# The first two chunks reordered, and layer norm's weight folded into W1: one change to a linear-attention, MLP and expert kernel

## The reference, cut to what matters

```python
for t in range(S):
    cur = np.einsum('bhd,bhe->bhde', u[None] * kt, vt)
    y[:, :, t] = np.einsum('bhd,bhde->bhe', rt, state + cur)
    state = w[None, :, :, None] * state + np.einsum('bhd,bhe->bhde', kt, vt)
```

```python
xn = (x - mu) / np.sqrt(var + 1e-06) * g_ln
ch = np.maximum(xn @ w_ch1, 0.0) @ w_ch2
return x + ch
```

## Time and profile before

| | us |
|---|---|
| median of 3 runs | 412.55 (412.34 to 412.64) |
| the profiled execution's own time | 412.14 |
| its span, first to last instruction | 410.3 |
| PE busy in the span | 399.5 (97%) |
| DVE, ACT, POOL busy | 227.3, 162.5, 120.1 |
| mean granted clock of TensorE | 0.987 of full speed |

### The profile page before, as it was taken

How to read it: one execution, slowest core, us unless ns; L and a number is a source line. 1 busy time by engine, 2 the same in 40 slices (tenths; PEclk the granted TensorE clock), 3 DMA queues, 4 the chain that set the end, 5 groups by cost and what they waited for, 6 DMA issues and landing times.

```text
span 410.3 us, 8140 instructions
## 1 busy us (share of the span) xinstructions
PE 399.5 (97%) x2761; PEld 369.4 (90%) x2761; DVE 227.3 (55%) x455; ACT 162.5 (40%) x300; POOL 120.1 (29%) x111
## 2 busy tenths in 40 slices
PE   8999999999999999999999999999999999999992
PEld 7999999999999999999999965679999999999982
DVE  7566954532542452344466856878853665638340
ACT  5456223232321321223234126356754672555530
POOL 2675280650162054000000400712331133114221
PEclk9699999999999999999999999999999999999998
DMA  7994310420330033140002848499894549111111
GB/s 225 344 290 125 104 40 6 143 79 19 99 106 19 19 102 102 45 149 2 19 22 64 285 137 287 147 314 313 291 371 155 180 129 370 66 30 41 27 41 41
DMA packets 32631, 54.87 MB, mean 134 GB/s; under 512 B 3261, under 2 KB 20323, under 8 KB 32592
## 3 DMA queue, kind: packets, MB, share of 16 engines
q1 hardware_dynamic: 30288, 48.07, 36.0%
q0 software_dynamic: 2304, 6.30, 5.0%
HBM read 49.64 MB, written 5.51 MB: 134 GB/s over the span
## 4 chain that ended last, share of the span: by engine, by line
PE 91%; DMA 3%; ACT 2%; DVE 1%; SPq 1%; issue 1%; POOL 0%; DVEq 0%; POOLq 0%
PE bank L940 6%; PE bank L856 6%; PE bank L857 6%; PE bank L858 6%; PE bank L942 6%; PE bank L946 6%; PE bank L894 5%; PE bank L1236 5%; PE bank L1208 5%; PE bank L1244 5%; PE bank L1240 5%; PE bank L1212 5%; PE bank L1215 5%; PE bank L1225 3%; PE bank L868 3%; PE bank L1137 3%
## 5 line engine op out<-in xcount | busy, mean ns | idle before, releaser
L652 ACT ACTIVATE parts<-bank 128x512 fp32r<-128x512 f32 x36 | 21.5, 597 | 85.1 <-PE bank L946 85.1
L1394 DVE SCALAR_TENSOR_TENSOR parts<-bank,parts 128x512 fp32r<-128x512 f32 x36 | 24.8, 690 | 45.2 <-ACT parts L652 45.1
L856 PE MATMUL bank<-parts 128*128 128x384 f32 x144 | 49.0, 341 | 0.0
L858 PE MATMUL bank<-parts 128*128 128x384 f32 x144 | 48.2, 335 | 0.0
L857 PE MATMUL bank<-parts 128*128 128x384 f32 x144 | 48.2, 334 | 0.0
L732 ACT ACTIVATE parts<-stage (+1 forms) x32 | 46.1, 1485 | 2.5 <-DMA stage<-in_w 2.3
L1702 DVE TENSOR_TENSOR parts<-stage,parts x24 | 41.1, 1756 | 5.3 <-ACT parts L732 4.5
L595 POOL DMA_INDIRECT out_y<-late x14 | 20.4, 1460 | 77.8 <-DVE late L1733 77.8
L940 PE MATMUL bank<-xnT_hi,parts 128*128 128x256 f32 x216 | 40.5, 296 | 0.5 <-DVE parts L1353 0.5
L942 PE MATMUL bank<-xnT_hi,parts 128*128 128x256 f32 x216 | 37.6, 283 | 0.0
L946 PE MATMUL bank<-xnT_lo,parts 128*128 128x256 f32 x216 | 37.6, 283 | 0.0
(11 more groups left out here) (239 smaller groups left out, 808.9 us busy)
## 6 DMA issues: line engine op xcount, KB each, us to landing
stage<-in_w SPq DMA_DIRECT2D x36, 768.0 KB, 7.5
stage<-in_w_ch SPq DMA_DIRECT2D x6, 768.0 KB, 9.3
arena<-in_k_t SPq DMA_DIRECT2D x12, 224.0 KB, 3.0
arena<-in_r_t SPq DMA_DIRECT2D x12, 224.0 KB, 2.9
arena<-in_k_rows SPq DMA_DIRECT2D x12, 192.0 KB, 2.8
arena<-in_v_rows SPq DMA_DIRECT2D x12, 192.0 KB, 3.4
x_rows<-stage SPq DMA_DIRECT2D x12, 192.0 KB, 1.9
arena<-in_r_rows SPq DMA_DIRECT2D x10, 192.0 KB, 2.6
```

Of the source, the lines that this page charges most:

```text
L652: act.activation(hT_hi[:, 2 * q:2 * q + 2, :].rearrange("p a t -> p (a t)"), bk[6 + q % 2][:], ACT.Relu).then_inc(h_hi_ready, 1)
L856: pe.matmul(out_, a_lo, b_hi, start=start, stop=False)
L858: return pe.matmul(out_, a_hi, b_hi, start=False, stop=stop)
L1394: dve.scalar_tensor_tensor(hT_lo[:, at, :].rearrange("p a t -> p (a t)"), bk[6 + q % 2][:], 0.0, hT_hi[:, at, :].rearrange("p a t -> p (a ...
```

## The change

Seven edits:

1. The decays of chunk 0 are made pair by pair (`decays_by_pair`): eight instructions of 128 columns instead of two of 512, each waiting only for the table of its own pair. `scores(0)` waits for one pair at a time, by the new semaphore `s_pair`.
2. The load of the first constants (identity and mask) is issued ahead of kT and rT of chunk 1, and on DVE `masked(0)` now stands ahead of chunk 1's decays (`second_decays`).
3. On TensorE `scores(1)` moves behind `from_scores(0)`, and matmuls on zeros are placed between the narrow ones: 2, 2, 4, 2 and 4 of them, where 16 stood in one block.
4. The factor -g_ln goes from `turned` into `round_piece` and `rest_of_piece` of pieces 0 to 2. Those now take three instructions each, one for a block of 128 features, and `turned` takes one instruction per chunk on ACT and one on DVE, in every group.
5. Piece 0's lo goes from POOL to DVE, ahead of `turned(0)`. `lo_p` is gone; everything counts on `lo_v`.
6. `ngcol` is made by POOL between `ends(0)` and `ends(1)`.
7. On ACT `centre(0)` and `turned(0)` move ahead of piece 1, and in group 0 every further piece comes one place later: piece 2 behind hidden 0, piece 3 behind hidden 1, piece 4 behind hidden 2, piece 5 behind the decay of chunk 3's state. The decay of chunk 2's state now stands ahead of piece 4.

```diff
@@ sync
             for u in range(2):
                 sp.dma_start(kT[u], k_t[u]).then_inc(s_turned[u], 16)
                 sp.dma_start(rT[u], r_t[u]).then_inc(s_turned[u], 16)
-            sp.dma_start(cst[:, 0:P + C], consts[:, 0:P + C]).then_inc(s_const, 16)
+                if u == 0:
+                    sp.dma_start(cst[:, 0:P + C], consts[:, 0:P + C]).then_inc(s_const, 16)
@@ gpsimd
             ends(0)
+            pool.wait_ge(s_g, 16)
+            pool.tensor_scalar(ngcol[:], gcol[:], -1.0, None, ALU.mult).then_inc(s_ng, 1)
             ends(1)
             diagonal(0)
-            pool.wait_ge(s_g, 16)
-            pool.tensor_scalar(ngcol[:], gcol[:], -1.0, None, ALU.mult).then_inc(s_ng, 1)
             diagonal(1)
-            first_piece(0)
-            first_piece(1)
@@ scalar
             def round_piece(i):
                 act.wait_ge(s_piece[i], 16)
-                act.activation(piece_at(i, 0), piece_stage(i), ACT.Copy).then_inc(hi_done, 1)
+                if i >= KD:
+                    act.activation(piece_at(i, 0), piece_stage(i), ACT.Copy).then_inc(hi_done, 1)
+                    return
+                if i == 0:
+                    act.wait_ge(s_ng, 1)
+                for k in range(KD):
+                    mm = act.activation(piece_at(i, 0)[:, k, :], piece_stage(i)[:, k, :], ACT.Copy, scale=ngcol[:, k:k + 1])
+                mm.then_inc(hi_done, 1)
...
-                    for k in range(KD):
-                        i = act.activation(xnT_hi[:, k, u * P:(u + 1) * P], bk[u][:, k * P:(k + 1) * P], ACT.Copy,
-                                           scale=ngcol[:, k:k + 1])
-                    i.then_inc(xnT_hi_ready, 1)
+                    act.activation(xnT_hi[:, :, u * P:(u + 1) * P],
+                                   bk[u][:, 0:DM].rearrange("p (k t) -> p k t", k=KD), ACT.Copy).then_inc(xnT_hi_ready, 1)
@@ tensor
             def scores(c, u, banks):
...
                 for p in range(NP_):
+                    if isinstance(c, int) and c == 0:
+                        pe.wait_ge(s_pair, p + 1)
...
             coefs(0, bk[3])
-            scores(1, 1, bk[6:8])
+            keep_warm(1, 5)
             for u in range(2):
                 pe.wait_ge(s_rows[u], R_FIRST)
             from_scores(0, 0, bk[4], scT[0], True)
+            keep_warm(1, 5)
+            scores(1, 1, bk[6:8])
             coefs(1, bk[0])
+            keep_warm(2, 5)
             from_scores(1, 1, bk[5], scT[1], True)
...
             gain(0, 0, bk[3])
+            keep_warm(1)
             turn_xn(0, lambda: gain(1, 1, bk[2]))
-            keep_warm(8)
+            keep_warm(2)
             pe.wait_ge(s_gw, 16)
@@ vector
+            def decays_by_pair():
+                dve.wait_ge(s_turned[0], T_LOADS)
+                for p in range(NP_):
+                    dve.wait_ge(s_wk, p + 1)
+                    k = dve.tensor_tensor(kT[0][:, p, :], kT[0][:, p, :], w_k[:, p, :], ALU.mult)
+                    if p == NP_ - 1:
+                        k.then_inc(kdec_ready, 1)
+                    dve.wait_ge(s_wr, p + 1)
+                    dve.tensor_tensor(rT[0][:, p, :], rT[0][:, p, :], w_r[:, p, :], ALU.mult).then_inc(s_pair, 1)
...
             def rest_of_piece(i):
                 dve.wait_ge(hi_done, i + 1)
...
+                for k in range(KD):
+                    x = dve.scalar_tensor_tensor(piece_at(i, 1)[:, k, :], piece_stage(i)[:, k, :], ngcol[:, k:k + 1],
+                                                 piece_at(i, 0)[:, k, :].bitcast(F32), ALU.mult, ALU.subtract)
+                x.then_inc(lo_v, 1)
...
-            first_decays(0)
+            decays_by_pair()
             raw_products(0)
-            first_decays(1)
             dve.wait_ge(s_const, 16)
             masked(0, bk[0:2], scT[0])
+            second_decays()
+            first_coefs(0, bk[3])
             raw_products(1)
-            first_coefs(0, bk[3])
...
             mean(0, 1)
-            dve.wait_ge(s_ng, 1)
+            rest_of_piece(0)
             turned(0)
             rest_of_piece(1)
```

More of the change, by code:

```diff
@@ L673, in group @@
                 if first:
-                    round_piece(3)
+                    round_piece(2)
                 else:
@@ L685, in group @@
                 if first:
-                    round_piece(5)
+                    round_piece(4)
                 hidden(g, range(3, 4))
                 decay(g * 2 + 3, 1)
+                if first:
+                    round_piece(5)
                 hidden(g, range(4, NHP))
@@ L711, in _ @@
             round_piece(0)
+            centre(0)
+            turned(0)
             round_piece(1)
-            centre(0)
-            act.wait_ge(s_ng, 1)
-            turned(0)
             act.wait_ge(s_eps, 1)
             deviation(0)
-            round_piece(2)
             group(0)
@@ L860, in scores @@
             def scores(c, u, banks):
-                pe.wait_ge(kdec_ready, c + 1)
-                pe.wait_ge(rdec_ready, c + 1)
+                if not isinstance(c, int) or c > 0:
+                    pe.wait_ge(kdec_ready, c + 1)
+                    pe.wait_ge(rdec_ready, c + 1)
                 if not isinstance(c, int) or c >= 2:
@@ L1384, in turned @@
                     at = slice(u * P, (u + 1) * P)
-                    for k in range(KD):
-                        i = dve.scalar_tensor_tensor(xnT_lo[:, k, at], bk[u][:, k * P:(k + 1) * P], ngcol[:, k:k + 1],
-                                                     xnT_hi[:, k, at].bitcast(F32), ALU.mult, ALU.subtract)
-                    i.then_inc(xnT_ready, 1)
+                    dve.tensor_tensor(xnT_lo[:, :, at], bk[u][:, 0:DM].rearrange("p (k t) -> p k t", k=KD),
+                                      xnT_hi[:, :, at].bitcast(F32), ALU.subtract).then_inc(xnT_ready, 1)
             def hidden(g, pairs):
```

47 lines of the change are left out of this document (18 added, 29 removed).

## The result

The changed kernel is slower. Its median of 6 runs is 418.75 us (417.75 to 420.17), against 412.44 (411.13 to 414.30) of the kernel before in 6 runs: ratio 1.0155, 95% interval 1.012 to 1.0191. The forecast was 411.15, with a range up to 412.6, and gave "slower" a chance of 0.15. It had the sign wrong.

The account below looks back on a forecast made before the run. TensorE, busy in 97% of the span, was taken as the bound. Gains of 0.9 us at `scores(2)` and 0.5 at q = 4 made -1.4, so 412.55 became 411.15; own range 410.7 to 411.6, full range 410.3 to 412.6.

Parts of the forecast that it names:

- 0.9 us at `scores(2)`: Chunk 2's scores on TensorE, behind POOL's two products, were to start at 26.0 instead of 26.88: -0.9 us.
- 0.5 at q = 4: In group 0, TensorE's 0.53 us wait for piece 2's lo was to go, with the state decay ahead of piece 4.
- just clear of 23.33: DVE's lo of piece 1 was to run from 21.3 to 23.2, before kT of chunk 2 lands at 23.33.
- paragraph on the clock: If the low stretch stays, hi is there at 21.6 and group 0 starts at 21.7: 0.2 us lost.
- POOL held again: Rival at POOL's first product for chunk 2: 2.01 us again, 0.7 of the gain goes, 411.85; chance 0.12.
- The first chunks gain nothing up to there.: Start-up: `from_scores(0)` at 9.55 instead of 10.70, the gain given back, x of chunk 1 at 16.4 to 16.6.
- It matters only if a half-speed stretch comes after 20.95: TensorE's clock ahead of group 0: half speed there was to cost only 0.2 us against the sum.
- The slower rival: Clock falls at 21 or later, after waits for `wg` and POOL; 6.8 us half speed, +1.4, 413.95; chance 0.14.
- What it set against itself: Against the slower case: at the trace's end TensorE idled from 402.5, the clock fell only at about 406.7.
- kT of chunk 2: Transfer that POOL's chunk 2 products wait for; taken to land at 23.33, as before the change.
- The start of group 0 that it forecast, 20.95: TensorE was to start group 0 behind router weights `wg`, landed at 20.93, instead of at 22.39.
- The fold costs nothing in the later groups: Cheaper `turned` runs under output matmuls while TensorE has no wait from 40 to 240 us: 0, with 0.1 either way.

Follow-up runs that it names:

- e2: Changed kernel with the fold taken back: a piece's hi and lo one instruction each, `turned` three; 415.57 us, ratio 1.0075.
- e7: Kernel before with only ACT's order in group 0 changed: decay of chunk 2's state ahead of piece 4, piece 5 later; 412.08 us, ratio 0.9998.
- e13: Changed kernel with chunk 1's scores and decays back in their old order and piece 1's hi early; 412.01 us, ratio 0.9993.
- e16: Changed kernel with piece 1's lo made in six instructions of 256 columns instead of three of 512; 422.06 us, ratio 1.0227.
- e1: Changed kernel with one wait added: POOL begins chunk 2 only when DVE has made piece 1's lo; 416.06 us, ratio 1.005.
- e4: Changed kernel with ACT rounding piece 1 ahead of `centre(0)`, as before the change; 416.52 us, ratio 1.0089.
- e6: Kernel before with edits 4 to 7 alone (fold, piece 0's lo on DVE, `ngcol` earlier, ACT's new order); 414.84 us, ratio 1.0041.
- e12: Kernel before with edits 4 to 7 alone, but ACT's hi of piece 1 ahead of `centre(0)`; 414.11 us, ratio 1.0005.
- e15: Kernel before with DVE's order alone changed: chunk 1's decays behind `masked(0)`, `first_coefs(0)` ahead of `raw_products(1)`; 418.82 us, ratio 1.0152.
- e14: Kernel before with one move on TensorE alone: `scores(1)` behind `from_scores(0)`; 414.45 us, ratio 1.0043.
- e10: Kernel before with edits 1 to 3, but the 16 zeros left in one block; 415.76 us, ratio 1.0066.
- e5: Kernel before with edits 1 to 3 alone (decays by pair, mask first, `scores(1)` later, zeros spread); 416.55 us, ratio 1.0076.
- e3: Changed kernel with 30 matmuls on zeros on TensorE behind chunk 2's scores, where it waited before q = 2; 419.08 us, ratio 1.0133.
- e8: Changed kernel with 48 instead of 14 matmuls on zeros in the first chunks; 418.3 us, ratio 1.0126.
- e9: Kernel before with only the zeros spread as in the change, nothing moved; 412.38 us, ratio 0.9992.

## Why the prediction was wrong

The forecast was added up from two gains, 0.9 us at `scores(2)` and 0.5 at q = 4, and had no term for a wait at q = 2. In the profiled execution `scores(2)` started at 26.69, which is 0.2 earlier than before, and not at 26.0.

**The step that failed first: piece 1's lo "just clear of 23.33".** The prediction took this lo from 21.3 to 23.2, and made 23.33, POOL's start, the point from which it costs something. But `round_piece(1)` stands on ACT behind the turned hi of chunk 1, and that was done at 22.1, not at 19.5: x of chunk 1 was 1.4 us late, and what followed it ran at half speed until 20.4. So ACT had the hi of piece 1 from 22.01 to 23.95, and DVE began at 23.98, when POOL already ran. The prediction's own paragraph on the clock had this case ("hi is there at 21.6") and carried it only to the start of group 0, 0.2 us, not to piece 1: 21.6 and 1.9 for ACT give a lo from 23.5 on, beside POOL. The margin was 0.13 us and the error 2.7.

**The price of that step, with the wrong sign of who waits.** The case "POOL held again" gave POOL 0.7 us more and the time 411.85. In after POOL was held for 0.3 to 0.5 us a product (1.75, 1.33 and 1.44 for 1.28, 1.00 and 1.00). But DVE was held for 3.3 (5.41 for 2.08), and TensorE waited 3.71 where the prediction saw no term at all. The Trainium skill (SBUF — State Buffer, "Who interferes with whom") says that the later of the two stands still. The traces agree, in both directions: L492 2.64 behind DVE in e2, DVE's three behind POOL here. What the prediction did not draw from it is that the rule holds for each instruction. The fold made one instruction into three, so the wait came up to three times; 2.58 us in one (e7), 3.74 in three at the same place (e13) and 7.14 in six (e16) confirm it. That the overlap is a cause of the loss is shown: with POOL held back (e1) or the fold undone (e2) the ratio is 1.005 and 1.0075, and both intervals lie below that of after. With the hi of piece 1 early it is 1.0089 (e4), whose interval just touches it. e6 and e12 point the same way: edits 4 to 7 alone cost 0.41% [0.1, 0.72], and with the hi of piece 1 back in its place 0.05% [-0.21, 0.32].

**"The first chunks gain nothing up to there."** The start of `from_scores(0)` moved from 10.70 to 10.85, not to 9.55, and x of chunk 1 came at 17.89 (forecast 16.4 to 16.6, before 16.41). Two things were missed. The 40 zeros of the start ended at 8.34 in this execution, not at 6.97, which put `scores(0)` 1.1 us later. And chunk 1's decays were moved from an empty stretch into the one in which POOL works on `k_end`; the prediction counted their 1.2 us as taken out of one place and at no price in the other. They took 1.45 and 0.68 in after, and the product behind them 1.30 for 0.69: 1.4 us more in all ahead of `masked(1)`. In e15 they took 1.47 and 1.48. Alone, that move costs 1.52% (e15), the move of `scores(1)` 0.43% (e14), both with the rest of edits 1 to 3 0.66 to 0.76% (e10, e5). The two are not additive. My reading, not tried by itself: with `scores(1)` behind `from_scores(0)`, TensorE has work while DVE makes the decays.

**The clock: "It matters only if a half-speed stretch comes after 20.95".** This step failed too. The prediction priced the low stretch ahead of group 0 at 0.2 us, and no term of its sum let that stretch grow. In the profiled execution the stretch even shrank to 3.4 us, and group 0 still started at 22.22, not at 20.95 or 21.7. But this was the execution with the least half-speed time of the six (13.3 us; the others 18.3 to 20.9, without a trace). In the traces of e1, e3, e4, e5, e10 and e16, all with edits 1 to 3, the stretch lasts 10.2 to 13.7 us, x of chunk 1 comes at 20.5 to 21.4 and group 0 starts at 26 to 27.1; e2 and e8 have no stretch. So in the profiled execution the whole loss lies behind the start of group 0, while in e5 and e10 it lies ahead of it. How the loss of the other five executions of after divides was not seen.

The slower rival named the right place and nearly the right length: half speed on dense work after 20.95. It had the fall at 21, behind waits for `wg` and POOL; the fall came at 30.6, behind a wait for DVE. What it set against itself from the earlier trace rows, over 4 us of idle time before a fall, did not carry over: here the clock fell 2.8 us after TensorE had run out of work at 27.8.

**What was right.** kT of chunk 2 let POOL start at 23.46 (forecast 23.33). The start of group 0 that it forecast, 20.95, was reached where the low stretch is short or absent (20.90 in e7, 20.91 in e2), but not in after. The wait at q = 4 goes with the decay ahead (e7). The fold costs nothing in the later groups: behind q = 4 the kernels differ by 0.1 us.

**What stays open.** The runs of one kernel differ by up to 7.4 us (e1: 411.63 to 419.04; 5.6 without its slowest), and within e1, e2, e5, e6, e13 and e14 the time goes up by 0.4 to 0.5 us for each us of half-speed time. It is not so everywhere: 0.6 in e12, 0.8 in e8, 0.2 to 0.3 in after, e4, e7, e9 and e15, and nothing in e10. That is a relation over runs, read from mean clocks; which event makes the clock fall in one run and not in the next was not found. Nor was it shown whether the fall at 30.6 goes when the wait of 3.71 goes: in e6 one of 3.4 us stands behind a wait of 2.23, in e16 one of 6.8 behind 5.26, and no run took the wait away with the rest as in after.

## What to carry to other kernels

Before a VectorE instruction with two SBUF inputs is split or moved, look up what GpSimd does in that stretch: each of the pieces can wait for one GpSimd instruction, so a split in three that costs 0.3 us alone (2.08 for 1.75) cost 1.2 there (3.74 for 2.58), and in the worst place the three lost 3.3 us. A step with a margin of 0.1 us against such an overlap belongs into the prediction as a case with the price of both sides waiting, and the price is read at the engine that TensorE waits for. Where a start-up is moved under a clock that varies, compare many runs: the one profiled execution may be the mildest. And a low stretch ahead of the dense work is no free stretch: here each start of group 0 after 23 came with 10 us of it or more.
